# Outer products of one chunk and scores of the next in one TensorE stretch, chunk loads reordered, and the last stores written as a loop

## The reference

```
state = alpha[t] * state + k[t] (outer) v[t]        # per batch and head, 48x48
y[t]  = q[t] @ state
x = y reshaped to 3072 x 384
x = (sigmoid(x @ w_gate) * (x @ w_val)) @ w_out     # width 1536
x = max(x @ w1, x @ w2, x @ w3) @ w_out2            # width 768
```

## Time and profile before

| what | value |
|---|---|
| median of 3 runs | 844.16 us (844.14 to 844.74) |
| profiled execution, its time | 844.45 us |
| its span | 842.7 us |
| PE busy | 833.3 us, 99% |
| DVE, ACT, POOL busy | 384.7, 274.8, 74.5 us |
| share of PE in the chain that ended last | 96% |
| granted TensorE clock | 1.0 (full, the 2.4 GHz level) |

### The profile page before, as it was taken

The page is one execution under the profiler, slowest core; times in us unless marked ns, Lnnn a source line. Parts: engine busy times, 40 slices in busy tenths (PEclk is TensorE's granted clock), DMA queues, the critical chain, the costliest instruction groups (busy, mean ns, idle before and its releaser), DMA issues.

```text
span 842.7 us, 15954 instructions
## 1 busy us (share of the span) xinstructions
PE 833.3 (99%) x6667; PEld 730.4 (87%) x6667; DVE 384.7 (46%) x932; ACT 274.8 (33%) x490; POOL 74.5 (9%) x68
## 2 busy tenths in 40 slices
PE   8999999999999999999999999999999999999998
PEld 7899999999999988788878888888888888888886
DVE  8787555556567656554653322323223232332321
ACT  4655333333333333334333333312212122221312
POOL 1000111111111101110210043100000000000000
PEclk9999999999999999999999999999999999999999
DMA  7441111111112211110112022000101001010101
GB/s 289 168 179 49 54 49 48 55 49 49 54 49 84 69 46 38 60 57 13 41 45 85 1 75 75 1 1 1 38 0 37 0 0 37 0 37 0 38 0 39
DMA packets 14271, 42.35 MB, mean 50 GB/s; under 512 B 1888, under 2 KB 5472, under 8 KB 14208
## 3 DMA queue, kind: packets, MB, share of 16 engines
q1 hardware_dynamic: 14144, 41.41, 14.0%
q10 hardware_dynamic: 64, 0.05, 0.0%
HBM read 35.56 MB, written 4.72 MB: 48 GB/s over the span
## 4 chain that ended last, share of the span: by engine, by line
PE 96%; DVE 2%; DMA 1%; issue 0%; ACT 0%; SPq 0%; DVEq 0%
PE ps_gv L1041 35%; PE ps_out L1065 19%; PE ps_gv L1047 18%; PE ps_out L1157 6%; PE ps_sc L1041 6%; PE ps_sc L1047 3%; PE ps_pair L1157 2%; PE ps_pair L1014 1%; PE ps_pair L995 1%; PE ps_pair L946 1%; PE ps_sc L966 1%; PE ps_sc L980 1%; PE ps_pair L966 0%; DVE rdec L714 0%; DVE decay L699 0%
## 5 line engine op out<-in xcount | busy, mean ns | idle before, releaser
L1041 PE MATMUL ps_gv<-x_hi,w_hi 128*128 128x512 f32 (+1 forms) x720 | 267.2, 371 | 1.4 <-ACT x_hi L473 1.4
L1041 PE MATMUL ps_gv<-x_hi,w_lo 128*128 128x512 f32 (+1 forms) x720 | 264.7, 368 | 0.0
L1047 PE MATMUL ps_gv<-x_lo,w_hi 128*128 128x512 f32 (+1 forms) x720 | 226.2, 368 | 0.0
L1041 PEld LDWEIGHTS ps_gv<-x_hi,w_hi 128*128 128x128 f32 x720 | 135.2, 188 | 17.7 <-issue 1.5
L1047 PEld LDWEIGHTS ps_gv<-x_lo,w_hi 128*128 128x128 f32 x720 | 133.8, 188 | 17.9
L1041 PEld LDWEIGHTS ps_gv<-x_hi,w_lo 128*128 128x128 f32 x720 | 135.3, 188 | 15.7
L813 DVE TENSOR_TENSOR h_sb<-act_sb,ps_gv 128x384 f32<-128x384 f32 (+1 forms) x84 | 51.2, 610 | 149.2 <-PE ps_gv L1047 149.2
L473 ACT ACTIVATE h_hi<-h_sb 128x384 fp32r<-128x384 f32 (+1 forms) x84 | 48.0, 571 | 146.5 <-DVE h_sb L813 146.1
L517 ACT ACTIVATE act_sb<-ps_gv 128x384 f32<-128x384 f32 (+1 forms) x84 | 45.1, 537 | 141.2 <-PE ps_gv L1047 141.2
L910 DVE TENSOR_TENSOR probs<-probs,ps_gv 128x512 f32<-128x512 f32 x36 | 24.7, 687 | 138.4 <-PE ps_gv L1047 138.4
L777 DVE TENSOR_TENSOR h_lo<-h_sb,h_hi 128x384 fp32r<-128x384 f32 (+1 forms) x84 | 51.7, 615 | 49.1 <-ACT h_hi L473 49.1
(11 more groups left out here) (128 smaller groups left out, 969.6 us busy)
## 6 DMA issues: line engine op xcount, KB each, us to landing
inbuf<-att_in SPq DMA_DIRECT2D x23, 704.0 KB, 4.5
mid<-w SPq DMA_DIRECT2D x12, 576.0 KB, 7.5
inbuf<-att_in SPq DMA_DIRECT2D x23, 256.0 KB, 2.8
inbuf<-w SPq DMA_DIRECT2D x6, 768.0 KB, 4.4
out<-inbuf SPq DMA_DIRECT2D x5, 768.0 KB, 3.5
out<-inbuf SPq DMA_DIRECT2D x4, 192.0 KB, 2.5
mid<-att_in SPq DMA_DIRECT2D x1, 704.0 KB, 8.9
x_raw<-x_raw SPq DMA_DIRECT2D x18, 32.0 KB, 1.9
```

The source lines that it names most:

```text
L1041: mm(bank, w_at(half, f, c + k * P, total=total), x_hi[:, k, 0:w], start=(k == 0 and half == 0), stop=False)
L1047: return mm(bank, w_at(0, f, c + k * P, total=total), x_lo[:, k, 0:w], start=False, stop=(k == KT - 1))
```

## The change

The tables of steps become one list of slots, `START_UP` and `SLOTS`. `SCORE`, `OUTER`, `ATTEND`, `ADD` and `SCAN` say what is done in which step. For chunks from 6 on (`JOINED`), the outer products of chunk C move from behind val of its own step to the step in which chunk C+1 is scored, ahead of those scores and behind the gate product; its values follow a step later. Outer products of these chunks go to other columns of the same banks. So slots have a distance of three steps, and four of them are in step 11: scores of chunk 6 at (tile 0, step 11), of 13 at (2, 11), of 17 at (3, 11) and of 21 at (4, 11). Chunks 6 to 22 give 17 joined stretches; the outer products of chunks 3, 4, 5 and 23 stand alone as before.

```
+START_UP = tuple((0, f) for f in (2, 5, 8))
+SLOTS = ((0, 11), (1, 2), (1, 5), (1, 8), (2, 2), (2, 5), (2, 8), (2, 11), (3, 2), (3, 5), (3, 8), (3, 11),
...
+SCORE = {at: C for C, at in enumerate(START_UP + SLOTS[:-1], PRO)}
+OUTER = {at: C for C, at in enumerate(START_UP + SLOTS[1:], PRO)}
+ATTEND = {shifted(at, 1): C for at, C in OUTER.items()}
+ADD = {(at if at[1] == 9 else shifted(at, 1)): C for at, C in ATTEND.items() if C >= JOINED}
+SCAN = {shifted(at, -2): C for at, C in SCORE.items() if C > PRO}
```

On PE (`y_taken` is the wait for `y_evac` and `y_added`), and on DVE:

```
                     product(ps_gate[:, 0:w], f, 0, W1C, ...).then_inc(gate_done, 1)
+                    if summed is not None and summed >= JOINED:
+                        outer(summed)
                     if scored is not None:
                         scores(scored)
                         transposes(scored)
...
 def outer(C):
                 pe.wait_ge(khs_done, C + 1)
-                if C >= PRO:
+                if C >= JOINED:
+                    y_taken(C)
+                    pe.wait_ge(state_done, states_by(C - 1))
...
 def attend(C):
+                    if JOINED <= C < CHUNKS - 1:
+                        pe.wait_ge(mask_done, 2 * C + 4)
+                        pe.wait_ge(khs_done, C + 2)
...
 dve:
                     if scanned is not None:
                         scans(scanned)
+                    if summed is not None and summed >= JOINED:
+                        if scored is not None:
+                            dve.wait_ge(sc_done, scored + 1)
+                        new_state(summed)
                     if scored is not None:
                         masked(scored, 0)
                         masked(scored, 1)
```

On SP, the load of alpha from chunk 5 on waits for `viol_done` alone, and that of q, k and v for `y_done`. The chunk loads stand one or two chunks further ahead of `move_last`. The stores become a loop of 192 KB pieces:

```
-            for T in range(TILES2 - 1):
-                sp.wait_ge(o_evac, T * SUB + SUB)
-                sp.dma_start(out[T], stage_out).then_inc(stored, 16)
-            for s in range(SUB):
-                sp.wait_ge(o_evac, (TILES2 - 1) * SUB + s + 1)
-                sp.dma_start(out[TILES2 - 1][:, s, :], stage_out[:, s, :]).then_inc(stored, 16)
+            with sp.Fori(0, TILES2) as T:
+                for s in range(SUB):
+                    sp.wait_ge(o_evac, T * SUB + s + 1)
+                    sp.dma_start(out[T][:, s, :], stage_out[:, s, :]).then_inc(stored, 16)
```

More of the change, by code:

```diff
@@ L406, in _ @@
             load_chunk(5)
-            for T in range(1, TILES - 1):
-                load_chunk(FIRST[T + 1])
+            load_chunk(6)
+            for T in range(1, TILES):
+                ahead = 1 if T <= 2 else 2
+                for C in range(FIRST[T + 1] + 1, FIRST[T + 1] + ahead):
+                    if C < CHUNKS:
+                        load_chunk(C)
                 move_last(T)
-                for C in range(FIRST[T + 1] + 1, FIRST[T + 2]):
-                    load_chunk(C)
-            move_last(TILES - 1)
+                if T + 2 <= TILES:
+                    for C in range(FIRST[T + 1] + ahead, FIRST[T + 2] + 1):
+                        if C < CHUNKS:
+                            load_chunk(C)
             for j in range(NF2):
@@ L801, in layer1 @@
                     g = T * NF1 + f
-                    scanned, scored, added = (chunk_at(T, f, steps) for steps in ("scan", "score", "add"))
-                    if scanned == PRO:
-                        scanned = None
+                    scanned, scored, summed, added = (plan.get((T, f)) for plan in (SCAN, SCORE, OUTER, ADD))
                     if scanned is not None:
                         scans(scanned)
+                    if summed is not None and summed >= JOINED:
+                        if scored is not None:
+                            dve.wait_ge(sc_done, scored + 1)
+                        new_state(summed)
                     if scored is not None:
@@ L1082, in layer1 @@
                     product(ps_gate[:, 0:w], f, 0, W1C, T * KT if f == 0 else None).then_inc(gate_done, 1)
-                    scored, attended = chunk_at(T, f, "score"), chunk_at(T, f - 1, "score")
+                    scored, summed, attended = (plan.get((T, f)) for plan in (SCORE, OUTER, ATTEND))
+                    if summed is not None and summed >= JOINED:
+                        outer(summed)
                     if scored is not None:
@@ L1091, in layer1 @@
                     product(ps_val[:, 0:w], f, DM, W1C).then_inc(val_done, 1)
-                    if scored is not None:
-                        outer(scored)
+                    if summed is not None and summed < JOINED:
+                        outer(summed)
                     if attended is not None:
```

74 lines of the change are left out of this document (41 added, 33 removed).

## The result

| what | before | after |
|---|---|---|
| median of the runs compared | 844.29 us (20 runs, 843.98 to 845.12) | 845.81 us (20 runs, 844.7 to 847.41) |
| profiled execution | 844.45 us | 846.42 us |
| its span | 842.7 us | 844.6 us |
| start of PE's last matmul | 838.41 us | 840.29 us |
| from there to the end of the span | 4.26 us | 4.33 us |

The ratio is 1.0018, with a 95% interval of 1.0011 to 1.0024. The change makes the kernel slower by 1.5 us, which is small but can be told from none. The runs after are also spread over 2.7 us, those before over 1.1.

The account below looks back on a forecast made before the run. PE, busy 833.3 of 842.7 us, was taken as the bound. From the profiled 844.45 us, -5.6 + 5.7 + 0.3 - 0.6 gave 844.25, less 0.29 for the median: 844.0 us, range 841.5 to 847.0.

Parts of the forecast that it names:

- Part 1: PE's 17 joined outer-product stretches lose their own entry and exit, 0.33 us each: -5.6 us.
- Rival B: A break between outer products and scores, so joined stretches save nothing: 849.6 us, chance 0.08.
- Part 2: At four tile ends ACT's `check` stands before the input splits of blocks 1 and 2, so PE waits: +5.7 us.
- DVE's fuller last step: Four state instructions and two masks ahead of h make it late at (3, 11): 0.1 us.
- Rival A: Tile ends don't stall, because ACT reaches the blocks earlier or PE's wait is covered: 838.3 us, chance 0.12.
- Part 3: Outer products of joined stretches wait on PE for `y_add` at 7 places, 5 before: +0.3 us.
- The prediction's own sign of being wrong: PE's waits outside the forecast places add up to more than 1 us, or the tile ends show none.
- Part 4: Loads issued only two steps ahead of use stay hidden from PE, with over 1 us to spare: 0.
- Rival C: q or k comes late at nine slots in tiles 1 to 3, costing 9 us: 853 us, chance 0.04.
- or of DVE with its fuller step, to 846 or 847: 0.06: Smaller waits for late q or k, or for DVE with more work in its step: 846 or 847 us, chance 0.06.
- Part 5: Last stores: in a loop SP has its code already, so the slow issue at the end goes: -0.6 us.

Follow-up runs that it names:

- experiment 1: Changed kernel with `check` of a chunk scored in step 11 put behind the splits of blocks 1 and 2: 840.92 us, ratio 0.9959.
- experiment 2: Changed kernel with `y_add` ahead of the low part of h on DVE, except in step 9: 844.03 us, ratio 0.9994.
- experiment 3: Changed kernel with both `check` behind the splits of blocks 1 and 2 and `y_add` ahead of the low part of h: 838.44 us, ratio 0.9929.
- experiment 4: Kernel before with one idle POOL multiplication (112x512) in the step ahead of scores of chunks 7 to 15: 846.26 us, ratio 1.0022.
- 11: Kernel before with one long idle POOL copy (112 x 1024) in the step ahead of the scores: 846.55 us, ratio 1.0022.
- 12: Kernel before with one long idle POOL multiplication (112 x 1024) in the step ahead of the scores: 852.23 us, ratio 1.009.
- experiment 6: Kernel before with the loop of stores alone: 844.63 us, ratio 1.0004.
- experiment 7: Kernel before with one idle POOL copy (one SBUF input, 0.61 us) in the step ahead of the scores: 844.49 us, ratio 1.0003.
- 9: Kernel before with three idle POOL copies in a row in the step ahead of the scores: 844.41 us, ratio 1.0001.
- 10: Kernel before with two idle POOL multiplications in a row in the step ahead of the scores: 846.63 us, ratio 1.0025.

## Why the prediction was right or wrong

**Part 1, right.** -5.6 forecast, -6.0 in the trace, 0.35 to 0.37 us a stretch, with no break between outer products and scores. Rival B is out. By the Trainium skill's rule (TensorEngine Tiling, Key Properties) TensorE drains where the tiling mode changes, not where the tile alone does; the 0.39 us between the first starts, with no drain between, agree with it.

**Part 2, right.** +5.7 forecast, 5.5 in the trace, 4.9 when `check` alone was moved (experiment 1, on medians that spread by over 1 us). The 0.1 us for DVE's fuller last step did not appear: tile 3 cost 1.45 against 1.43 in tile 2. Rival A is out.

**Part 3, wrong, and this is the step that made the kernel slower:** without these waits experiment 2 is at 0.9994 of the kernel before. "Now the outer products of the joined stretch wait for the same `y_add`": the seven places are right, and the price was not. I took 0.15 us each, the wait of the earlier trace rows, as if the end of `y_add` stayed where it was. It moved: what stands in front of `y_add` on DVE, the low part of h, is held by POOL. +2.1 us in place of +0.3. The prediction's own sign of being wrong, over 1 us of waits outside its places, has come.

**Part 4, wrong in the question it asked.** "Hidden, with over 1 us to spare" holds for q and k as PE sees them: only 0.13 us at (2, 8) in this trace, though experiment 3 has 0.4 at one slot. But I costed the load only to the moment at which PE needs its result. The POOL work that the landing releases changed its place: ahead of the landing's move it ran at 110.95, in a step where nothing of DVE's was near PE. The earlier trace rows had the two durations, and the trace before has `y_add` directly behind the low part (119.36, behind 118.88). The clue was there: PE already waited 0.15 us for that chain. The hold itself stands in the trace before too, once for each of the chunks 6 to 23. DVE's eight scans of `recips` (L714) read alpha and `zero`, both in SBUF, and POOL's first piece of k starts among them:

```profile
97.95 2.51 DVE L714 TENSOR_TENSOR_SCAN rdec<-inbuf,rdec,zero 112x63 f32<-112x63 f32 x8
...
99.10 0.74 POOL L445 TENSOR_TENSOR inbuf<-inbuf,rdec 112x256 f32<-112x256 f32 x1 [1.84 <-DVE rdec L714]
```

The one scan due just behind POOL's start, at 99.17, lasts 0.80 us where the median is 0.32, and the eight take 2.51 us; in the change, at 116.41, with no POOL beside them, they take 2.03. Rival C, with "or of DVE with its fuller step, to 846 or 847: 0.06", names the right engine and time, with the wrong cause; experiment 4 made the cost with DVE's step unchanged.

The rule that I overlooked stands in the Trainium skill (SBUF — State Buffer, section "SBUF: two separate sides"): DVE and GpSimd share a pair of ports to SBUF as an exclusive lock, and a DVE operation with two SBUF inputs and a GpSimd operation that reads SBUF block each other for the whole instruction, whichever starts first. This case's traces agree: the low part ends 0.42 us after POOL's instruction in seven slots and in experiments 4, 11 and 12; POOL's next instruction waits in its turn (1.05 us instead of 0.74), and where DVE started first POOL was held: in the change, DVE's split of a weight (L795, two operands in SBUF) runs from 85.54 for 1.32 us, and the piece of k that POOL starts at 85.70 takes 1.77 us; `h_sb`, which reads one operand from PSUM, keeps 0.55 us beside POOL (186.52 beside a POOL instruction from 186.24).

**Part 5, wrong.** -0.6 forecast, 0 in the trace. "In a loop SP executes code that it has already" was argued from one packet beside one slow issue. The loop has the packet and the slow issue too (1.10 us), so has the form written out, and the loop alone gained nothing (experiment 6). The Trainium skill (Runtime: NRT & Kernel Launch, Instruction fetch mechanics) calls the crossing of a block of code mostly hidden. Here the slow issue beside such a packet takes 0.74 to 1.38 us instead of 0.33 to 0.45; if the packet is SP's code, which no run shows, it is not hidden.

**The sum.** Parts 1 and 2 were off by -0.4 and -0.2, parts 3 and 4 by +1.8, part 5 by +0.7, and the start-up, not forecast, by +0.2. That is +2.1 us, and 844.25 + 2.1 = 846.35, against 846.42 in the profiled execution. That the miss stayed this small is in part luck: the first two errors took 0.6 us off the others.

## What to carry to other kernels

When a load is moved, price not only the wait for it but the work that its landing releases: on which engine it will run, at what moment, and what the neighbour that shares SBUF's port pair with it is doing then. An instruction that can be held should have nothing urgent behind it: the order of two independent instructions on DVE was worth 1.8 us here, and with `check` behind the splits the joining's 6 us came out whole. A wait of 0.15 us on the critical path is a warning: whatever delays its chain goes through one to one.

## What the runs showed of the hardware that I had not expected

- DVE's operation with two SBUF operands ends 0.40 to 0.43 us after the POOL instruction that ran when it was due, for POOL instructions of 0.61 to 1.89 us, with one operand or two (experiments 4, 7, 11, 12 and seven slots). As it takes 0.56 us by itself, a POOL instruction that ended 0.08 us after its start cost it nothing (experiment 7, 119.17 against 119.09).
- DVE gets its turn between two POOL instructions issued in a row; the second is the one that waits (experiments 9 and 10: POOL's mean 701 against 612 ns, 1138 against 1043; in the change, a piece of k of 1.05 against 0.74 us). A DVE instruction that starts first holds POOL as well (0.74 us became 1.77 beside a split of 1.32, at 85.70 in the change).
- A POOL copy of 112 x 1024 takes 1.04 us and one of 112 x 512 0.61 us; a multiplication takes 1.04 us for 512 columns where both operands are the same, and 1.29 us in the kernel's own use with two different ones. Why the same operand is cheaper was not tried.
- A DMA issue on SP takes 0.33 to 0.45 us in the last stores. One of the four takes longer in every trace, 0.65 us (experiment 1) to 1.38 (experiment 3), in a loop and in straight code, and ends 0.2 to 0.4 us after an instruction packet; not every issue beside such a packet does (experiment 2 has one of 0.33 us at 837.81, inside the packet of 837.68 to 838.94).
